# A fused attention, MLP and expert kernel: the second MLP matrix is split by GpSimd during the attention and kept in DRAM; the hash products and their transfers are regrouped

## Chip, cores and metric

The kernel runs on one core of one Trainium2 chip. The metric is the device time of one execution in microseconds (us). All arrays are float32 in DRAM.

## The reference

```python
# attention: 2 batches, 8 heads, 768 rows, head size 64; proj is 64 x 6
q_bits = (q @ proj > 0);  k_bits = (k @ proj > 0)              # 6 hash bits per row
mask   = bucket(q_bits)[:, None] == bucket(k_bits)[None, :]     # same bucket
scores = where(mask, q @ k.T / 8, -1e9)
attn   = exp(scores - max) / (sum + 1e-9);   x = attn @ v       # x: 1536 x 512
# MLP: w_in 512 x 2048, w_out 2048 x 512
h = x @ w_in
g = (a0 + a1 h + a2 h^2 + a3 h^3) / (1 + |b0||h| + |b1| h^2 + 1e-6)
x = g @ w_out
# experts: 8 of 512 -> 1024 -> 512; each row goes to its argmax expert
out[row] = gate * sigmoid_gate * (relu(x @ w1[e]) @ w2[e])
```

## The kernel before

There are 16 attention heads, worked off one after the other in six steps each (one step is 128 query rows); `PAIRS` = 8 loop turns hold two heads each, `par` 0 and 1, and buffers with two copies are indexed by `par`. Every engine has its own instruction stream, written out by hand, and the streams meet in semaphores. The steps of TensorE are in `step` (L515): it turns q and k of a head two ahead (`turn_qk`, L449, into the PSUM bank `ps_p`), multiplies them with the hash matrix (`hash_qk`, L462, into the same bank), computes scores for two steps ahead (`scores`, L470), transposes probabilities (`turn_probs`, L487) and multiplies them with v (`attend`, L499).

The mask is made by extra rows of the score product. `hash_qk` gives the projections and their negatives; VectorE compares and scales them (`mask_rows`, L1009, 128 x 384 into `mask_st`); SyncE copies 12 rows at a time from `mask_st` into rows 64 to 75 of `q_mask` and `k_mask` (`place_masks`, L293, four transfers for a head). The bank `ps_p` is free for the next `turn_qk` only when `mask_rows` has read it.

Products keep float32 accuracy by splitting each operand into a high part in the TensorE type float32r and a low part, and by three products (high-high, high-low, low-high). For q and k GpSimd makes the high part `qkT_hi` (L1347) and the low parts (L1354, L1360), and SyncE places the high part four times (`place_hi`, L287). GpSimd also splits one 128-column piece of `w_in` for each head (`split_win`, L1391), scales the attention output by the inverse row sums (L1381), which come back from DRAM as a broadcast row (`load_scale`, L312), and makes its low part (`lo_of_x`, L1383).

SyncE issues all transfers of the attention in the order of `attention_head` (L335): masks, inverse sums out, v, inverse sums in, a piece of `w_in`, q and k, x into `xT`, high parts. It waits before each one (`hold`, L258), so an issue that has to wait holds up all behind it.

The MLP has four groups of 384 rows and in each 16 pieces f of the 2048 hidden columns. TensorE alternates `mlp_up` (L577, 12 products) and `mlp_down` (L587, 9 products), three pieces apart; ScalarE and VectorE work out g between them, GpSimd its low part (L1460). In the first group there is more to do. `w_out` comes in 16 pieces of 128 x 512 into three buffers `x2_sb` (`load_wout`, L367); ScalarE makes the high part (`hi_of_wout`, L867), VectorE the low part (`lo_of_wout`, L1132), 16 pieces over the first ten steps (`TAIL` = 10), and each later load waits for a low part (L390). At step 4 ScalarE waits for the last transfers of x (L906), since `wout_hi` and `wout_lo` lie over buffers of the attention. The tile pool of the attention and that of the MLP share one stretch of SBUF.

After the MLP the rows are routed to experts, and 19 slots of 128 rows go through the expert matrices, which ScalarE, VectorE and GpSimd split in the same way.

## Time and profile before

| | us |
|---|---|
| median of 3 runs (821.36 to 823.01) | 822.98 |
| profiled execution, its own time | 822.91 |
| span of its trace, first to last instruction | 820.9 |
| TensorE busy | 785.3 (96%) |
| VectorE busy | 662.0 (81%) |
| ScalarE busy | 589.6 (72%) |
| GpSimd busy | 347.6 (42%) |

In the trace the attention lies from 0 to about 255 us, the MLP from 256 to about 550, the routing to about 575 and the experts to the end. PE is TensorE, PEld its weight loads, DVE is VectorE, ACT ScalarE, POOL GpSimd, SP SyncE. A busy TensorE need not be at its peak, since the ends of its products are modelled. "L583" is line 583 of the kernel. The column of the granted clock reads 1.00 for 2.4 GHz and 0.50 for 1.2 GHz.

### The profile page before, as it was taken

To read this page: it belongs to the slowest core of one execution; us is meant where nothing else is said; L and a number is where in the kernel's file an instruction comes from. 1 tells how busy PE (TensorE), PEld (TensorE's weight loads), DVE (VectorE), ACT (ScalarE), POOL (GpSimd) and SP (SyncE) were. 2 spreads that over 40 slices of the span, in tenths; PEclk is the share of its full clock that TensorE was granted. 3 is DMA by queue.
4 is the path that set the end of the run, shared out by engine and by line. 5 is a ranking of instruction groups with operands and counts; after the bars stand their busy time and mean duration, and the time that the engine had idled before them with its cause. 6 is when DMAs were issued, how large, how long until landed. Compare 5 with 4: busy or idle time off the path is not lost.

```text
span 820.9 us, 16572 instructions
## 1 busy us (share of the span) xinstructions
PE 785.3 (96%) x5050; PEld 678.1 (83%) x5050; DVE 662.0 (81%) x1101; ACT 589.6 (72%) x1046; POOL 347.6 (42%) x319
## 2 busy tenths in 40 slices
PE   8999999999998799999999999996999999999995
PEld 6888888888887688999899999976788888888884
DVE  5777777777785899788877878767899999999982
ACT  5666766767666688776676777642799988988973
POOL 5365565564643213222222222211356765565452
PEclk9999999999999999999999999997899999999999
DMA  5666786786644320100010010044782113516930
GB/s 128 141 149 159 164 180 145 174 179 146 157 98 117 109 77 2 39 1 0 0 38 0 0 38 0 1 142 165 273 288 80 38 51 111 170 45 213 373 124 1
DMA packets 75236, 88.64 MB, mean 108 GB/s; under 512 B 34355, under 2 KB 51459, under 8 KB 75204
## 3 DMA queue, kind: packets, MB, share of 16 engines
q1 hardware_dynamic: 72004, 80.11, 35.6%
q0 software_dynamic: 3040, 8.13, 3.0%
q8 instruction: 17, 0.28, 0.1%
q14 instruction: 15, 0.12, 0.1%
q10 hardware_dynamic: 160, 0.00, 0.0%
HBM read 108.82 MB, written 8.18 MB: 143 GB/s over the span
## 4 chain that ended last, share of the span: by engine, by line
PE 85%; DVE 7%; ACT 2%; issue 2%; DMA 2%; POOL 1%; DVEq 0%; SPq 0%; POOLq 0%; ACTq 0%
PE ps_s L583 14%; PE ps_t L751 13%; PE ps_s L728 13%; PE ps_t L601 9%; PE ps_o L510 9%; PE ps_t L496 7%; PE ps_o L601 4%; PE ps_s L481 4%; PE ps_s L483 3%; PE ps_s L737 2%; PE ps_p L459 2%; PE ps_p L466 1%; DVE mask_st L1014 1%; PE ps_o L715 1%; PE ps_p L642 1%
## 5 line engine op out<-in xcount | busy, mean ns | idle before, releaser
L1460 POOL TENSOR_TENSOR g_lo<-num_b,g_hi 128x384 fp32r<-128x384 f32 x64 | 65.8, 1028 | 217.3 <-ACT g_hi L875 128.1
L583 PE MATMUL ps_s<-xT,win_hi 128*128 (+1 forms) x512 | 133.0, 340 | 0.0
L1019 DVE TENSOR_REDUCE row_max<-ps_s 128x1 f32<-128x768 f32 x96 | 91.0, 948 | 44.9 <-PE ps_s L483 44.8
L1296 DVE TENSOR_TENSOR w_lo<-w_raw,w_hi 128x1024 fp32r<-128x1024 f32 x76 | 124.9, 1701 | 2.3 <-ACT w_hi L930 0.6
L795 ACT ACTIVATE probs<-ps_s,exp_bias,exp_scale 128x768 f32<-128x768 f32 x96 | 95.4, 993 | 9.1 <-DVE exp_bias L1031 8.9
L583 PEld LDWEIGHTS ps_s<-xT,win_hi 128*128 128x128 f32 x512 | 92.7, 189 | 3.8 <-issue 0.3
L801 ACT ACTIVATE probsT<-ps_t 128x384 f32<-128x384 f32 x96 | 47.3, 492 | 60.4 <-PE ps_t L496 60.4
L583 PE MATMUL ps_s<-xT,win_lo 128*128 (+1 forms) x256 | 86.2, 337 | 0.0
L496 PE MATMUL ps_t<-ident,probs 128*128 128x128 f32 x576 | 80.3, 276 | 0.9 <-DVE probsT L1045 0.9
L510 PE MATMUL ps_o<-probsT,v_raw 128*64 128x128 f32 x1152 | 76.3, 277 | 1.9 <-DVE probsT L1045 1.9
L930 ACT ACTIVATE w_hi<-w_raw 128x1024 fp32r<-128x1024 f32 x76 | 76.5, 1062 | 0.8 <-DMA w_raw<-in_moe_w_dram 0.6
L510 PEld LDWEIGHTS ps_o<-probsT,v_raw 128*64 128x64 f32 x1152 | 62.8, 137 | 16.9 <-issue 12.0
L938 ACT ACTIVATE w_hi<-w_raw 128x1024 fp32r<-128x1024 f32 x76 | 75.0, 1062 | 1.7 <-DMA w_raw<-in_moe_w_dram 1.6
L481 PE MATMUL ps_s<-k_mask,q_mask 76*128 76x384 f32 x192 | 73.8, 384 | 1.4 <-ACT qkT L790 0.9
L496 PEld LDWEIGHTS ps_t<-ident,probs 128*128 128x128 f32 x576 | 65.3, 140 | 8.1 <-issue 4.1
L1304 DVE TENSOR_TENSOR w_lo<-w_raw,w_hi 128x1024 fp32r<-128x1024 f32 x57 | 66.2, 1212 | 5.6 <-ACT w_hi L938 5.4
L1123 DVE SCALAR_TENSOR_TENSOR num_b<-num_b,coef,den_b 128x384 f32<-128x384 f32 x64 | 40.2, 629 | 32.9 <-ACT den_b L865 31.2
L483 PE MATMUL ps_s<-k_cross,q_cross 128*128 128x384 f32 x192 | 65.3, 340 | 0.0
L728 PE MATMUL ps_s<-w_hi,xgT_hi 128*128 128x512 f32 x152 | 61.7, 406 | 1.7 <-DVE xgT_lo L1309 1.7
L751 PE MATMUL ps_t<-w_hi,hT_hi 128*128 128x512 f32 x152 | 60.7, 399 | 1.2 <-issue 1.2
L1045 DVE COPY probsT<-ps_t 128x384 f32<-128x384 f32 x96 | 52.9, 551 | 9.9 <-PE ps_t L496 8.5
L728 PE MATMUL ps_s<-w_hi,xgT_lo 128*128 128x512 f32 x152 | 60.0, 395 | 0.0
(210 smaller groups left out, 1959.6 us busy)
## 6 DMA issues: line engine op xcount, KB each, us to landing
w_raw<-in_moe_w_dram SPq DMA_DIRECT2D x152, 512.0 KB
xT<-x_st SPq DMA_DIRECT2D x32, 192.0 KB, 3.7
scale_row<-row_inverse_scratch SPq DMA_DIRECT2D x32, 191.8 KB, 3.7
win_raw<-in_moe_w_in_dram SPq DMA_DIRECT2D x16, 256.0 KB, 3.9
x_sb<-in_moe_w_out_dram SPq DMA_DIRECT2D x16, 256.0 KB, 2.8
qk_raw<-in_q_dram SPq DMA_DIRECT2D x16, 192.0 KB, 3.2
qk_raw<-in_k_dram SPq DMA_DIRECT2D x16, 192.0 KB, 3.8
v_raw<-in_v_dram SPq DMA_DIRECT2D x16, 192.0 KB, 3.3
```

The lines of the kernel that those rows point to most:

```text
L481: pe.matmul(ps_s[slot][:, hb, 0:HALF], q_mask[par][0:KR, j * P:(j + 1) * P], k_mask[par][0:KR, cols], start=True, stop=False)
L483: mm = pe.matmul(ps_s[slot][:, hb, 0:HALF], q_cross[par][:, j * P:(j + 1) * P], k_cross[par][:, cols], start=False, stop=True)
L496: mm = pe.transpose(ps_t[hb][:, t * P:(t + 1) * P], probs[c % 2][:, col:col + P], ident[:])
L510: mm = pe.matmul(ps_o[g * D:(g + 1) * D, b * P:(b + 1) * P], v_raw[par][:, t, :], probsT[(QT * par + 2 * b + g) % 4][:, t, :], start=(t == ...
L583: mm = pe.matmul(h_bank[f % 4], a[w], xT[:, c, blocks, l, :], start=(c == 0 and n == 0), stop=(c == CD - 1 and n == 2))
L601: mm = pe.matmul(acc_bank[m][:], a[:, rows], b[:, f, :], start=(f == 0 and n == 0), stop=(f == NF - 1 and n == 2))
L728: mm = pe.matmul(h_slot[b], x[:, c, :], w[par][:, c, cols], start=(c == 0 and n == 0), stop=(c == CD - 1 and n == 2))
L751: mm = pe.matmul(y_ps[:], a[:, f, :], b[:, f, :], start=(f == 0 and n == 0), stop=(f == NE - 1 and n == 2))
L795: act.activation(probs[c % 2][:].rearrange("p (b n) -> p b n", b=2), ps_s[c % 2][:, :, 0:HALF], ACT.Exp, bias=exp_bias[:, c:c + 1], scale= ...
L930: act.activation(w1_hi[par][:, c, :], w1_raw[:, c, :], ACT.Copy).then_inc(w1_hi_made, 1)
L1019: dve.tensor_reduce(row_max[:, c:c + 1], ps_s[c % 2][:, :, 0:HALF], AX.XY, ALU.max).then_inc(maxed, 1)
L1296: dve.tensor_tensor(w1_lo[par][:, c, :], w1_raw[:, c, :], w1_hi[par][:, c, :].bitcast(F32), ALU.subtract).then_inc(w1_lo_made, 1)
```

## The change

Four edits.

- `w_out` is split during the attention. For each head SyncE loads one piece (`wout_raw`), GpSimd makes both parts (`split_wout`, at the end of its share of a head, before `lo_of_x`), and SyncE stores them, 512 KB, into a DRAM scratch. `hi_of_wout` and `lo_of_wout` are gone, and with them ScalarE's wait at step 4. SyncE loads the split pieces (512 KB each) into one tile `wout`: 0 and 1 when all scores are made, 2 to 5 after the place of the 15th head's x, 6 to 15 when all of x has been placed. `mlp_down` waits for piece f.
- The hash products of all heads but the first use a matrix of 32 columns and four groups of columns of the array, each on a quarter (192) of the rows. `mask_rows` then works on 128 x 192.
- The masks go through DRAM: one transfer out of `mask_st`, a wait until it has landed, and two transfers back (instead of four).
- The high part of k is placed into `k_mask` and `k_cross` by one transfer, since both now lie in one tile `k_both` (three transfers instead of four).

The first head keeps its own matrix `first_w` and its thresholds, so VectorE has more small instructions at the start.

```diff
@@ SyncE
+            def load_wout_raw(f):
+                sp.dma_start(wout_raw[:], wout_rows[f]).then_inc(wout_raw_in, 16)
+            def store_wout(f):
+                sp.dma_start(wout_dram[f], wout_st[:].bitcast(F32)).then_inc(wout_out, 16)
             def place_hi(par):
                 hi = qkT_hi[:].bitcast(F32)
-                for target, rows, part in ((k_mask, slice(0, D), slice(D, P)), (q_mask, slice(0, D), slice(0, D)),
-                                           (k_cross, slice(0, D), slice(D, P)), (q_cross, slice(D, P), slice(0, D))):
-                    sp.dma_start(target[par][rows, :].bitcast(F32), hi[part, :]).then_inc(hi_in[par], 16)
+                sp.dma_start(k_both[par][0:D, :, :].bitcast(F32),
+                             hi[D:P, :].unsqueeze(1).to_broadcast([D, 2, S])).then_inc(hi_in[par], 16)
+                for target, rows in ((q_mask, slice(0, D)), (q_cross, slice(D, P))):
+                    sp.dma_start(target[par][rows, :].bitcast(F32), hi[0:D, :]).then_inc(hi_in[par], 16)
+            def store_masks(par):
+                sp.dma_start(mask_dram[par], mask_st[:]).then_inc(mask_out, 16)
             def place_masks(par):
-                for hb in range(2):
-                    cols = slice(hb * HALF, (hb + 1) * HALF)
-                    for target, row in ((q_mask, HC * hb), (k_mask, HC * hb + ZK)):
-                        sp.dma_start(target[par][D:KR, cols].bitcast(F32),
-                                     mask_st[row:row + MR, :]).then_inc(mask_in[par], 16)
+                quarters = mask_dram[par].rearrange("(g r) n -> r g n", r=HQ)
+                for target, row in ((q_mask, 0), (k_mask, MR)):
+                    sp.dma_start(target[par][D:KR, :].bitcast(F32).rearrange("r (g n) -> r g n", n=QUARTER),
+                                 quarters[row:row + MR, :, :]).then_inc(mask_in[par], 16)
...
                     if more or par == 0:
                         hold(sp, masked, m + 2)
+                        store_masks(1 - par)
+                    if m0 > 1:
+                        hold(sp, wout_split, m - 1)
+                        store_wout(m - 2)
+                    load_wout_raw(m - 1)
+                    if more or par == 0:
+                        hold(sp, mask_out, 16 * (m + 1))
                         hold(sp, scored, QT * m)
                         place_masks(1 - par)
...
             def load_wout(f):
-                sp.dma_start(x2_sb[f % GT][:], wout_rows[f]).then_inc(wout_in[f % GT], 16)
+                sp.wait_ge(wout_out, 16 * (f + 1))
+                sp.dma_start(wout[:, f, :, :].bitcast(F32), wout_dram[f]).then_inc(wout_in[f], 16)
...
-            for f in range(GT):
+            sp.wait_ge(wout_split, NF - 1)
+            store_wout(NF - 2)
+            load_wout_raw(NF - 1)
+            sp.wait_ge(scored, QT * HEADS)
+            for f in range(2):
                 load_wout(f)
             sp.wait_ge(inverted, HEADS)
             store_inverse(1)
...
             load_scale(1)
+            sp.wait_ge(x_lo_made, START + HEADS - 1)
+            place_x(PAIRS - 1, 0)
+            for f in range(2, 6):
+                load_wout(f)
+            sp.wait_ge(wout_split, NF)
+            store_wout(NF - 1)
+            sp.wait_ge(x_lo_made, START + HEADS)
+            place_x(PAIRS - 1, 1)
+            sp.wait_ge(attended, BLOCKS * HEADS)
             for par in range(2):
-                sp.wait_ge(x_lo_made, START + HEADS - 1 + par)
-                place_x(PAIRS - 1, par)
-            for f in range(GT, NF):
-                sp.wait_ge(wout_lo_made, f - GT + 1)
+                sp.wait_ge(x_out[par], 16 * START + 32 * PAIRS)
+            sp.wait_ge(wout_out, 16 * NF)
+            for f in range(6, NF):
                 load_wout(f)
@@ TensorE
             def hash_qk(i, par):
                 pe.wait_ge(qk_copied, 4 * i + 2 * par + 2)
-                for hb in range(2):
-                    mm = pe.matmul(ps_p[HC * hb:HC * (hb + 1), 0:HALF], hash_w[:],
-                                   qkT[:, hb * HALF:(hb + 1) * HALF], start=True, stop=True)
+                for g in range(4):
+                    mm = pe.matmul(ps_p[HQ * g:HQ * (g + 1), 0:QUARTER], hash_w[:],
+                                   qkT[:, g * QUARTER:(g + 1) * QUARTER], start=True, stop=True)
                 mm.then_inc(hashed, 1)
...
-                pe.wait_ge(wout_lo_made, f + 1)
+                pe.wait_ge(wout_in[f], 16)
@@ ScalarE (mlp_step; hi_of_wout is gone)
-                if first:
-                    if f == 1:
-                        x_hi(PAIRS - 1, 1)
-                    if f == 4:
-                        for par in range(2):
-                            act.wait_ge(x_out[par], 16 * START + 32 * PAIRS)
-                    for b in range(NF * f // TAIL, NF * (f + 1) // TAIL):
-                        hi_of_wout(b)
+                if first and f == 1:
+                    x_hi(PAIRS - 1, 1)
@@ VectorE (lo_of_wout is gone)
-                dve.tensor_scalar(mask_st[:], ps_p[:, 0:HALF], hash_thr[:, 2:3], hash_thr[:, 3:4],
+                    dve.wait_ge(mask_out, 16 * (2 * i + par - 1))
+                dve.tensor_scalar(mask_st[:], ps_p[:, 0:QUARTER], hash_thr[:, 2:3], hash_thr[:, 3:4],
                                   ALU.is_ge, ALU.mult).then_inc(masked, 1)
@@ GpSimd
+            def split_wout(i, par):
+                n = 2 * i + par
+                pool.wait_ge(wout_raw_in, 16 * (n + 1))
+                if n > 0:
+                    pool.wait_ge(wout_out, 16 * n)
+                pool.tensor_scalar(wout_st[:, 0, :], wout_raw[:], 1.0, 0.0, ALU.mult, ALU.add).then_inc(wout_hi_made, 1)
+                pool.wait_ge(wout_hi_made, n + 1)
+                pool.tensor_tensor(wout_st[:, 1, :], wout_raw[:], wout_st[:, 0, :].bitcast(F32),
+                                   ALU.subtract).then_inc(wout_split, 1)
...
                     add_eps(i, par)
+                split_wout(i, par)
                 if 2 * i + par > 0:
                     lo_of_x(*done)
```

## Rows read from the trace of the kernel before

**Rows 1.** The page: the chain that ended last, by engine.
```profile
PE 85%; DVE 7%; ACT 2%; issue 2%; DMA 2%; POOL 1%; DVEq 0%; SPq 0%; POOLq 0%; ACTq 0%
```

**Rows 2.** Windows, a steady MLP stretch: length, busy by engine, clock, DMA share, GB/s.
```profile
350.00:400.00 50.00, 50.00 (x269) 45.55 (x268) 40.36 (x73) 34.64 (x72) 11.21 (x11) 1.00 0.00 0
```

**Rows 3.** Windows, one attention head of the loop.
```profile
98.19:113.33 15.14, 14.94 (x144) 12.64 (x146) 11.33 (x27) 10.51 (x23) 8.86 (x8) 1.00 0.71 166
```

**Rows 4.** Chain of waits within that head: start, length, what.
```profile
99.65 0.37 PE ps_s L481
100.02 0.18 PE ps_s L483
...
102.25 0.80 PE ps_p L466 x4
...
104.69 0.68 DVE mask_st L1014
```

**Rows 5.** Instruction groups by shape, 60 to 180 us: busy, mean ns, idle before.
```profile
L1399 POOL TENSOR_TENSOR win_lo<-win_raw,win_hi 128x512 fp32r<-128x512 f32 x8 | 10.3, 1294 | 0.7
...
L1025 DVE TENSOR_SCALAR exp_scale<-row_max 128x1 f32<-128x1 f32 x48 | 7.4, 154 | 1.7
...
L1014 DVE TENSOR_SCALAR mask_st<-ps_p,hash_thr 128x384 f32<-128x384 f32 x7 | 4.7, 669 | 0.0
```

**Rows 6.** Waits of the whole execution: us, times, longest.
```profile
PE ps_p L459 <- DVE mask_st L1014: 3.6, 14, 0.9
```

**Rows 7.** Waits of SyncE, 83 to 174 us (six heads).
```profile
SPq L261 <- PE ps_p L459: 6.9, 6, 1.6
```

**Rows 8.** Timeline of SyncE in that head: start, length, what.
```profile
106.40 0.65 SPq L291 DMA_DIRECT2D q_cross<-qkT_hi  x1
...
107.77 0.83 SPq L297 DMA_DIRECT2D q_mask<-mask_st  x1
...
110.21 0.71 SPq L297 DMA_DIRECT2D k_mask<-mask_st  x1
```

**Rows 9.** DMA issues of the whole execution: KB each, median us to landing.
```profile
x_sb<-in_moe_w_out_dram SPq DMA_DIRECT2D x16, 256.0 KB, 2.8
...
q_cross<-qkT_hi SPq DMA_DIRECT2D x15, 192.0 KB, 4.3
...
row_inverse_scratch<-row_inv SPq DMA_DIRECT2D x16, 3.0 KB, 1.6
```

**Rows 10.** Windows of 1 us, in that head and just before the MLP.
```profile
111.00:112.00 1.00, 1.00 (x12) 0.91 (x9) 0.85 (x4) 0.26 (x1) 0.00 (x0) 1.00 0.09 20
254.00:255.00 1.00, 0.78 (x7) 0.64 (x7) 0.30 (x2) 0.34 (x1) 0.00 (x0) 1.00 1.03 381
```

**Rows 11.** Timeline of GpSimd in that head.
```profile
114.71 1.01 POOL L1387 TENSOR_TENSOR x_st<-x_raw,x_st 128x384 fp32r<-128x384 f32 x1 [4.94 <-ACT x_st L812]
```

**Rows 12.** Timeline of TensorE in the first MLP group.
```profile
265.73 0.34 PE L583 MATMUL ps_s<-xT,win_lo 128*128 128x384 f32 x1
267.70 0.47 PE L601 MATMUL ps_t<-wout_hi,g_hi 128*128 128x512 f32 x1 [1.63 <-issue]
...
309.35 0.47 PE L601 MATMUL ps_t<-wout_hi,g_hi 128*128 128x512 f32 x1 [1.94 <-issue]
...
315.14 0.39 PE L601 MATMUL ps_t<-wout_hi,g_hi 128*128 128x512 f32 x1
```

**Rows 13.** Timeline of ScalarE at the same place.
```profile
264.86 1.16 ACT L870 ACTIVATE wout_hi<-x_sb 128x512 fp32r<-128x512 f32 x2
...
273.76 0.63 ACT L870 ACTIVATE wout_hi<-x_sb 128x512 fp32r<-128x512 f32 x1 [4.87 <-DMA x_sb<-in_moe_w_out_dram]
```

**Rows 14.** Timeline of GpSimd at the same place.
```profile
261.36 1.46 POOL L1381 TENSOR_TENSOR x_raw<-x_raw,scale_row 128x384 f32<-128x384 f32 x1 [4.20 <-DMA scale_row<-row_inverse_scratch]
```

**Rows 15.** Chain of waits in the steady MLP.
```profile
394.58 1.39 PE ps_t L601 x6
...
398.76 1.39 PE ps_t L601 x6
```

More of the change, by code:

```diff
@@ L97, in fused_kernel @@
                 row_inv = sb("row_inv", [P, STEPS])
-                k_cross = [sb(f"k_cross{i}", [P, S], F32R) for i in range(2)]
+                wout_raw = sb("wout_raw", [P, DM])
+                wout_st = sb("wout_st", [P, 2, DM], F32R)
                 v_raw = [sb(f"v_raw{i}", [P, QT, D]) for i in range(2)]
@@ L598, in mlp_down @@
                     rows = slice(m * P, (m + 1) * P)
-                    for n, (a, b) in enumerate(((g_hi[f % 4], wout_hi), (g_hi[f % 4], wout_lo),
-                                                (g_lo[f % 2], wout_hi))):
-                        mm = pe.matmul(acc_bank[m][:], a[:, rows], b[:, f, :], start=(f == 0 and n == 0),
+                    for n, (a, l) in enumerate(((g_hi[f % 4], 0), (g_hi[f % 4], 1), (g_lo[f % 2], 0))):
+                        mm = pe.matmul(acc_bank[m][:], a[:, rows], wout[:, f, l, :], start=(f == 0 and n == 0),
                                        stop=(f == NF - 1 and n == 2))
@@ L1003, in mask_first @@
                         rows = slice(row, row + MR)
[L1004 to L1006 removed]
+                        dve.tensor_scalar(target[0][D:KR, cols], ps_p[rows, 0:HALF], first_thr[rows, 2:3],
+                                          first_thr[rows, 3:4], ALU.is_ge, ALU.mult).then_inc(mask_in[0], 8)
+                dve.wait_ge(mask_in[0], 32)
                 dve.sem_inc(masked, 1)
@@ new lines, in _ @@
+            dve.tensor_scalar(hash_thr[0:HQ, 5:6], iota_p[0:HQ, :], float(MR), -BIG, ALU.is_ge, ALU.mult).then_inc(thr_made, 1)
+            dve.wait_ge(thr_made, 4)
+            dve.tensor_tensor(hash_thr[0:HQ, 2:3], hash_thr[0:HQ, 0:1], hash_thr[0:HQ, 1:2], ALU.add).then_inc(thr_made, 1)
+            dve.tensor_tensor(hash_thr[0:HQ, 3:4], hash_thr[0:HQ, 4:5], hash_thr[0:HQ, 5:6], ALU.add).then_inc(thr_made, 1)
+            dve.wait_ge(thr_made, 6)
+            for g in range(1, 4):
+                dve.tensor_copy(hash_thr[HQ * g:HQ * (g + 1), 2:4], hash_thr[0:HQ, 2:4]).then_inc(thr_made, 1)
@@ L1156, in mlp_step @@
                 from_hidden(g, f)
-                if first:
-                    for b in range(NF * f // TAIL, NF * (f + 1) // TAIL):
-                        lo_of_wout(b)
                 if not first and f in (4, 6, 8):
```

106 lines of the change are left out of this document (60 added, 46 removed).

## The prediction

> **What bounds the kernel now.** I read the page first: the chain that ended last runs through TensorE for 85% of the span, and TensorE is busy for 96% of it by the table [rows 1]. So an edit pays where TensorE waits, or where it takes work off TensorE. Next the windows, to see where it waits: in the steady MLP there is no idle time at all (50.00 of 50.00 us) and the DMA engines are at rest [rows 2]; nothing of the change touches that stretch. A head of the attention takes 15.14 us, TensorE is busy for 14.94 of them and the DMA engines for 71% [rows 3]: 0.20 us are to be had there, and the transfers have less room than any compute engine. Then the chain inside a head, to see what the 0.20 us are: the last non-TensorE piece of any length is the mask instruction on VectorE, 0.68 us, for which the next transposes into `ps_p` wait [rows 4]. Last, the first MLP group: only there does TensorE stand still for long.
>
> **Part 1: masks, VectorE.** The mask instruction took 669 ns on 128 x 384, and a tensor_scalar on 128 x 1 took 154 [rows 5]. Linear between them, 128 x 192 takes 154 + 192/384 x 515 = 412 ns, 0.26 us less, which is more than the 0.20 us that TensorE waits. All its waits for the mask are 3.6 us in 14 times [rows 6]; the longest, 0.9, is at the start and keeps about 0.6. Gain: 3.6 - 0.6 = 3.0 us.
>
> **Part 2: hash products, TensorE.** Four products' records (two halves, two passes each) take 0.80 us of the chain [rows 4]. They are now eight of half the length in four column groups. No row shows four groups at once, so I bound it. If all four stream together, the 0.64 us of pure streaming (4 x 384 columns at two cycles and 2.4 GHz, halved by the two groups; an estimate that fits the 0.80) becomes 0.32. If only two at a time do, nothing is saved. Against it stands a change of shape: the first score product after products with 64 columns takes 0.37 us in the chain, the next 0.18 [rows 4], so a change of the array's column split costs about 0.19 us. Before, the hash and the attention products behind it had the same 64 columns; now 32 meet 64, one such change more. Per head -0.32 + 0.19 = -0.13 to +0.19 us, for 15 heads -2.0 to +2.9. I take 0, near the middle, as no row is nearer to either end.
> The Trainium skill, TensorEngine Tiling (Array Packing), Key Properties, says that a change of tiling mode drains the engine while a change of tile does not, and its Theoretical Speedup gives up to four times for 32 columns. The 0.37 against 0.18 agrees with the first; the second no row here shows. By the speedup alone the sum would be 2 us lower, by the drain alone 2.9 higher.
>
> **Part 3: SyncE's queue in the attention.** Every transfer of a head hangs in one ordered queue. In six heads SyncE waited 6.9 us for TensorE's q/k transposes [rows 7], so it is spare for 1.15 us in each, and 0.95 once TensorE's head is 0.20 shorter. Gone are one issue of high parts, 0.65, and the four of masks, from 107.77 to 110.21 + 0.71 = 110.92, 3.15 us [rows 8]. New are three issues (masks out, split pair out, raw piece in), each between nearly nothing and the 0.83 of the dearest mask issue [rows 8], and a wait until the masks have landed in DRAM. Landing took 1.6 us for the 3 KB of inverse sums and 4.3 us for a high part behind three others [rows 9]. The mask store stands behind three high parts, so I take 3.3, and the other two issues lie inside it. Then two placements, 2 x 0.78. Sum: -0.65 - 3.15 + 3.3 + 1.56 = +1.06 us for a head, against 0.95 spare: SyncE would slip about 0.1 a head, 1.5 us over 14 heads. Ends: 1.6 gives -0.64, no slip; 4.3 gives +2.06, a slip of 1.1.
> A slip is hidden until it uses up the masks' lead. They are now issued by about 107.1 + 3.3 + 1.6 = 112.0 and land some 2 to 3 us later; the scores that need them stand just before the hash products, which come at 102.25 [rows 4] and one head later at 117.2, so at about 116.4. That is 1.4 to 2.4 us of lead, and a slip of 1.5 is just covered. I take off 0.5 for what is not.
> The data itself, 512 KB out and 256 KB in for a head, falls where the DMA engines now rest: they are 9% busy from 111 to 112 us [rows 10]. At the 381 GB/s of the wide raw pieces [rows 10] they are 2.1 us of data, and with the small pieces of the rest the engines' 71% [rows 3] become about 86%: it fits, with little left.
> The Trainium skill, DMA: Bandwidth & Descriptors, Anatomy of one DMA, puts most of about 2.0 us fixed cost on the receipt of the write. The 1.6 us for 3 KB is near it. By 2.0 instead of 3.3 SyncE would not slip, and the 0.5 would be gone.
>
> **Part 4: GpSimd.** The split adds a pair like that of `w_in`: 1.29 us for the subtraction [rows 5] and about half of that for the high part, 1.9 us. In each head GpSimd stood idle for 4.94 us before `lo_of_x` [rows 11], exactly where the pair is put; the raw piece, issued by about 109, should be there by 113, so the pair ends near 115 against 114.71. Behind the pair on GpSimd wait `lo_of_x` and the next head's high part, and for these SyncE's placements. By the spare time (4.94 - 1.9 = 3.0 us a head) the cost is 0; were the piece 3 us late, SyncE's queue would be late by what exceeds it.
>
> **Part 5: the first MLP group.** This is the large term. Before, `mlp_down` 0 starts at 267.70, 8 at 309.35, 9 at 315.14 [rows 12]. In between stand 16 high parts on ScalarE, 16 low parts on VectorE, ScalarE's wait for x and a raw piece, 4.87 us before 273.76 [rows 13], and a last raw piece before 309.35. All this goes. Then the group runs at TensorE's pace, one `mlp_down` after the other in 398.76 - 394.58 = 4.18 us [rows 15]; ScalarE is busy for 69% of such a stretch and VectorE for 81% [rows 2], so they keep up.
> The first `mlp_down`: one high part of `w_out` before the first logarithm and two (1.16 us [rows 13]) before g's high part fall away, about 1.3 us in the sum of both engines. TensorE itself is done with its four `mlp_up` at 265.73 + 0.34 = 266.07 [rows 12]. 267.70 - 1.3 = 266.4, held down by that to 266.3 at best; I take 266.3. The ninth after it starts at 266.3 + 9 x 4.18 = 303.9, against 315.14: 11.2 us. From the tenth on nothing is different.
> What is late next: the factors for the last head's x. GpSimd waited 4.20 us for them, to 261.36 [rows 14]; now 1.8 MB (a split pair out, a raw piece, two split pieces in) go into the queue ahead of them, against 0.77 MB before, 1.0 MB or 2.7 us more at 381 GB/s [rows 10], of which some 0.7 fall before the inverse sums are asked for. That puts them 2.0 us later, at 263.4; x is scaled 1.2 to 1.5 us later, at 264.7, and ScalarE asks for it at about 264.2. I take off 0.5. The split pieces 2 to 5 are there by 267, 6 to 15 are asked for at about 272 and come one in under 3 us, while TensorE needs number 6 at 266.3 + 6 x 4.18 = 291.4: hidden. TensorE's wait for all of x, at step 10, is 30 us away.
> The start: VectorE's additional small instructions lie in its waits for q, k and the constants. Cost 0, at most 0.4.
>
> **Sum.** -3.0 + 0.5 (masks and queue) + 0 (hash) - 11.2 + 0.5 = -13.2 us. Against the profiled execution's own 822.91 (its span is 820.9) that is 809.7; its time is within 0.1 us of the median 822.98. Forecast 809.7.
>
> **Rivals.**
> *A: the hash groups stream all at once and SyncE never slips.* For it: the landing of 1.6 us. Against: no row shows four groups. -3.0 - 2.0 - 11.2 = -16.2, so 806.7.
> *B: SyncE's queue sets the head in part.* Masks land in 3.8 us or issues cost 0.1 more each; slip 0.5 to 0.8 a head, less the lead of 1.7: 14 x 0.65 - 1.7 = 7.4 us back. With the two large gains, -3.0 - 11.2 + 7.4 = -6.8, about 816. For it: [rows 3, 7]; against: fewer small transfers in the DMA queue.
> *C: the queue turns the whole change over.* One mechanism: the wait for the masks in DRAM, with 512 KB and 256 KB behind it, makes SyncE's round longer than TensorE's head. It decides from a head of 15.14 + 11.0/14 = 15.9 us on, which is a round 1.0 us above TensorE's 14.94. With 4.3 us to landing, dear issues (0.83 each, within the wait) and the inverse sums' round trip longer by 0.7, a head takes 16.5: 14 x 1.36 - 11 = +8, so 831. Against: it needs all ends at once.
> *D: the first group gives half.* The factors or a split piece come 5 us late; ScalarE stands at step 1 or TensorE at an early `mlp_down`: 815. For it: the queue of 1.8 MB. Against: the lead of pieces.
> *E: the change does nothing, since the stall was TensorE's own.* [rows 12, 13] speak against; 823.
>
> **Chances.** Forecast 45% (its own range 807.5 to 812), A 17%, B 17%, C 8%, D 10%, E 3%. Range with both unknown ends: 805.5 to 818. What this kernel's measurement can tell from no change is about 0.2% (1.6 us). Faster: forecast, A, B, D, 89%, less 1 for their tails: 0.88; same 0.03; slower 0.09.
>
> **What would show it.** Head length: 14.9 to 15.0 right, above 15.14 B or C, and then TensorE waits for mask or high-part transfers at the first score product of a head. No wait for the mask instruction. The hash block in the chain: 0.55 to 0.7 is A, about 0.95 the drain alone. The tenth `mlp_down` 37.6 us after the first. No idle time of ScalarE for x in steps 1 to 4. What would make it wrong most cheaply: a mask store that lands more than 4 us after its issue.

## The result and the profile after

| | before | after |
|---|---|---|
| median of 6 runs each, interleaved, us | 822.62 (821.06 to 823.56) | 827.59 (826.19 to 828.24) |
| ratio after to before, 95% interval | | 1.0062 (1.0048 to 1.0076) |
| profiled execution, its own time | 822.91 | 828.0 |
| span | 820.9 | 826.2 |
| first `mlp_up` product starts | 255.80 | 265.93 |
| first `mlp_down` | 267.70 | 278.73 |
| tenth `mlp_down` | 315.14 | 317.91 |

The kernel became 0.62% slower where 1.6% faster was forecast. Between the two spans lie 5.3 us. The last three lines split them: the attention costs +10.13 (265.93 - 255.80). From the first `mlp_up` to the tenth `mlp_down` it is 51.98 us instead of 59.34, -7.36. Behind that nothing was expected, and +2.5 are there.

The page after: busy time by engine, the chain by engine, and the queue of SyncE's transfers (packets, MB, share of 16 engines).
```profile
PE 785.6 (95%) x5110; PEld 677.9 (82%) x5110; DVE 651.0 (79%) x1099; ACT 581.5 (70%) x1030; POOL 377.0 (46%) x351
...
q1 hardware_dynamic: 78892, 98.36, 42.2%
...
PE 73%; DMA 9%; SPq 8%; DVE 3%; issue 3%; ACT 1%; POOL 1%; POOLq 0%; DVEq 0%
```
TensorE's work is what it was (785.6 against 785.3 us), but its share of the chain fell from 85% [rows 1] to 73%, and DMA and SyncE's queue now hold 17%, where they had 2%. That is the first thing to see: the bound has moved to SyncE's ordered queue.

Two windows after: an early head (between two starts of `mask_rows`) and one of the middle.
```profile
72.67:87.42 14.75, 14.74 (x147) 12.51 (x147) 11.23 (x27) 10.51 (x23) 9.74 (x11) 1.00 0.85 206
103.53:119.66 16.13, 15.01 (x147) 12.55 (x147) 11.32 (x27) 10.51 (x23) 10.83 (x11) 1.00 0.92 207
```
A head takes 14.75 us up to the fifth, 0.39 less than before [rows 3], with TensorE busy throughout. From the sixth on the heads take 16.11, 16.13, 17.6, 15.38, 16.52, 16.36, 16.26, 19.45 and 14.75 us, and TensorE stands for 1.12 us in the one shown.

The chain inside such a head (start, length, what):
```profile
107.15 1.50 SPq L308
...
109.21 4.35 DMA hash_mask_scratch<-mask_st
...
114.19 1.91 DMA k_both<-hash_mask_scratch
116.09 0.34 issue
116.44 0.44 PE ps_s L531
...
117.40 0.46 PE ps_p L507 x8
```
TensorE's first score product waits for the placed mask, that for the mask in DRAM, and that for SyncE, which stood in the high part of q. Here is SyncE's round in the same head (start, length of the issue, what); it answers to [rows 8]:
```profile
105.85 0.60 SPq L305 DMA_DIRECT2D k_both<-qkT_hi  x1
106.50 0.60 SPq L308 DMA_DIRECT2D q_mask<-qkT_hi  x1
107.15 1.50 SPq L308 DMA_DIRECT2D q_cross<-qkT_hi  x1
109.21 0.34 SPq L311 DMA_DIRECT2D hash_mask_scratch<-mask_st  x1
109.91 0.46 SPq L301 DMA_DIRECT2D wout_split_scratch<-wout_st  x1
110.58 0.34 SPq L298 DMA_DIRECT2D wout_raw<-in_moe_w_out_dram  x1
113.82 0.31 SPq L316 DMA_DIRECT2D q_mask<-hash_mask_scratch  x1
114.19 0.36 SPq L316 DMA_DIRECT2D k_both<-hash_mask_scratch  x1
114.66 0.34 SPq L328 DMA_DIRECT2D row_inverse_scratch<-row_inv  x1
...
116.74 1.13 SPq L333 DMA_DIRECT2D scale_row<-row_inverse_scratch  x2
...
122.62 0.61 SPq L305 DMA_DIRECT2D k_both<-qkT_hi  x1
```
From 110.92 to 113.82 SyncE does nothing but wait. Through nearly all of this wait the DMA engines are full; they run low behind it, at the inverse sums (last two columns: DMA share, GB/s):
```profile
112.00:113.00 1.00, 1.00 (x20) 1.00 (x22) 0.93 (x4) 1.00 (x4) 0.00 (x0) 1.00 1.04 376
115.00:116.00 1.00, 0.31 (x3) 0.07 (x1) 0.93 (x4) 0.84 (x3) 0.62 (x1) 1.00 0.19 41
```
The round, from one high part of k to the next, is 16.77 us. For comparison the same four points of SyncE's round in the trace of before, where this one is 15.57 us (the rounds around it make up a mean head of 15.14):
```profile
104.44 0.50 SPq L291 DMA_DIRECT2D k_mask<-qkT_hi  x1
...
111.14 0.35 SPq L309 DMA_DIRECT2D row_inverse_scratch<-row_inv  x1
...
112.97 1.15 SPq L314 DMA_DIRECT2D scale_row<-row_inverse_scratch  x2
...
120.01 0.50 SPq L291 DMA_DIRECT2D k_mask<-qkT_hi  x1
```
After, the waits of SyncE over the attention (83 to 260 us: us, times, longest):
```profile
SPq L271 <- DMA hash_mask_scratch<-mask_st: 22.0, 10, 2.5
SPq L271 <- DMA row_inverse_scratch<-row_inv: 14.2, 12, 2.3
```
The wait for TensorE's transposes [rows 7] is gone: from 83 to 230 us SyncE waits for a compute engine only once, for 0.6 us (GpSimd), so it is practically never early any more. The landing times (KB, median us), for [rows 9]:
```profile
wout_split_scratch<-wout_st SPq DMA_DIRECT2D x16, 512.0 KB, 4.7
...
row_inverse_scratch<-row_inv SPq DMA_DIRECT2D x16, 3.0 KB, 1.9
...
q_cross<-qkT_hi SPq DMA_DIRECT2D x15, 192.0 KB, 5.9
```

The chain at the start of the MLP, which answers to [rows 12 to 14]:
```profile
265.59 4.49 DMA row_inverse_scratch<-row_inv
...
270.62 4.11 DMA scale_row<-row_inverse_scratch
...
274.87 1.63 POOL x_raw L1426
...
278.73 2.90 PE ps_t L650 x6
```
The factors of the last head come 13.5 us later than before (274.87 against 261.36), 3.4 of them beyond the 10.1 of the attention, and the first six products of `mlp_down` take 2.90 us instead of the 1.39 of [rows 15]. The windows say why (the column before the last two is the granted clock): 0.61 and 0.54, so about half of full speed (1.2 GHz), after TensorE had stood for 2.51 us before 278.73. Before the change it had stood there for 1.63 [rows 12] and ran on at 1.00.
```profile
278.00:280.00 2.00, 1.27 (x3) 1.11 (x4) 1.45 (x2) 1.93 (x4) 1.59 (x2) 0.61 1.03 354
280.00:282.00 2.00, 2.00 (x6) 1.52 (x6) 1.97 (x5) 0.84 (x2) 0.14 (x1) 0.54 0.98 330
```

### The profile page after: what moved, and what is told of

Read it like the earlier page. It is cut to its first block, busy times and chain, and to the rows that moved or that the text cites. A ratio compares the mean times of both kernels' runs of the same rounds, so it can differ in the third digit from the quotient of the medians.

```text
span 826.2 us, 16797 instructions
## 1 busy us (share of the span) xinstructions
PE 785.6 (95%) x5110; PEld 677.9 (82%) x5110; DVE 651.0 (79%) x1099; ACT 581.5 (70%) x1030; POOL 377.0 (46%) x351
## 4 chain that ended last, share of the span: by engine, by line
PE 73%; DMA 9%; SPq 8%; DVE 3%; issue 3%; ACT 1%; POOL 1%; POOLq 0%; DVEq 0%
PE ps_s L633 15%; PE ps_t L799 13%; PE ps_s L776 13%; PE ps_t L650 10%; PE ps_o L650 5%; DMA hash_mask_scratch<-mask_st 4%; PE ps_o L560 4%; PE ps_t L546 3%; DMA row_inverse_scratch<-row_inv 2%; SPq L308 2%; PE ps_s L531 2%; PE ps_s L785 2%; PE ps_s L533 2%; SPq L324 2%; PE ps_o L763 1%
## 5 line engine op out<-in xcount | busy, mean ns | idle before, releaser
L531 PE MATMUL ps_s<-k_both,q_mask 76*128 76x384 f32 x192 | 74.5, 388 | 12.3 <-DMA k_both<-hash_mask_scratch 9.3
L650 PE MATMUL ps_t<-wout,g_hi 128*128 128x512 f32 x248 | 78.1, 396 | 2.5 <-issue 2.5
L560 PE MATMUL ps_o<-probsT,v_raw 128*64 128x128 f32 x1152 | 78.0, 281 | 1.9 <-DVE probsT L1082 1.9
L533 PE MATMUL ps_s<-k_both,q_cross 128*128 128x384 f32 x192 | 65.6, 341 | 0.0
L902 ACT ACTIVATE den_b<-ps_s 128x384 f32<-128x384 f32 x64 | 31.3, 488 | 48.0 <-PE ps_s L633 47.8
```

What stands on the lines that cost most here:

```text
L531: pe.matmul(ps_s[slot][:, hb, 0:HALF], q_mask[par][0:KR, j * P:(j + 1) * P], k_mask[par][0:KR, cols], start=True, stop=False)
L533: mm = pe.matmul(ps_s[slot][:, hb, 0:HALF], q_cross[par][:, j * P:(j + 1) * P], k_cross[par][:, cols], start=False, stop=True)
L560: mm = pe.matmul(ps_o[g * D:(g + 1) * D, b * P:(b + 1) * P], v_raw[par][:, t, :], probsT[(QT * par + 2 * b + g) % 4][:, t, :], start=(t == ...
L650: mm = pe.matmul(acc_bank[m][:], a[:, rows], wout[:, f, l, :], start=(f == 0 and n == 0), stop=(f == NF - 1 and n == 2))
```

## The experiments

Theory Q: SyncE's round is one serial chain, and a DRAM write that is waited for lands only when the burst issued ahead of it (high parts, the 512 KB pair) has drained; the order of the transfers makes the head 16 us. Rival V: the added bytes alone do it, whatever the order. Rival P: it matters which queue issues. The expectations of the later runs call theory Q by the letter D. Times are medians; every kernel was compared with the kernel before in the same runs (there 822.3 to 822.8), and the ratio is to it.

**1. masks_only**: the masks through DRAM, the hash and `k_both`; `w_out` as before.
```diff
-                    if m0 > 1:
-                        hold(sp, wout_split, m - 1)
-                        store_wout(m - 2)
-                    load_wout_raw(m - 1)
```


> The hash, mask and high-part edits alone; w_out is split in the MLP as before. Theory Q (SyncE's round is one chain of issues and two DRAM round trips, and its length is the head): without the pair's issues and bytes ahead of them the masks land in about 3 us instead of 4.1 and SyncE fits; a head takes 14.74 us, as the first four heads of the changed kernel do, and the time is about 822.6 - 15 x 0.40 = 816.6. Theory V (the bytes of the split pair fill the DMA engines): the same, 816.6. If a head is above 15.1 here, the mask round trip alone is enough to lose.


Measured: 829.99, ratio 1.0111 (1.0080 to 1.0142). Heads 14.7 to 14.8 at first, then 15.3 to 17.8. The SyncE waits from 83 to 230 us:
```profile
SPq L269 <- DMA hash_mask_scratch<-mask_st: 34.5, 9, 5.6
SPq L269 <- DMA row_inverse_scratch<-row_inv: 6.6, 10, 1.3
```
Two issues of one round, and the DMA engines in between (last two columns: busy share, GB/s):
```profile
111.15 0.35 SPq L303 DMA_DIRECT2D hash_mask_scratch<-mask_st  x1
115.80 0.32 SPq L308 DMA_DIRECT2D q_mask<-hash_mask_scratch  x1
```
```profile
112.00:113.00 1.00, 1.00 (x9) 0.98 (x8) 0.52 (x2) 0.75 (x2) 0.00 (x0) 1.00 1.04 206
...
114.00:115.00 1.00, 1.00 (x21) 0.83 (x17) 0.78 (x3) 1.00 (x4) 0.04 (x1) 1.00 0.24 65
115.00:116.00 1.00, 1.00 (x9) 0.96 (x8) 0.03 (x1) 0.85 (x2) 0.96 (x1) 1.00 0.00 0
```
While the mask write is outstanding, the engines first work off the high parts at a share of 1.0 and then run empty, since SyncE issues nothing from 111.50 to 115.80. In this round burst and gap follow each other. The pair is not here at all, so its bytes are not needed for the loss; the DMA share from 83 to 230 us is 0.77, hardly above the 0.76 of before. Both theories had 816.6 for this run, and both missed it by 13 us: Q had let the masks land in about 3 us, and they took 4.3 (median).

**2. wout_only**: the pair through DRAM, the masks, hash and high parts as before (the diff's other edits undone).
```diff
+                    if m0 > 1:
+                        hold(sp, wout_split, m - 1)
+                        store_wout(m - 2)
+                    load_wout_raw(m - 1)
                     if more or par == 0:
                         hold(sp, masked, m + 2)
                         hold(sp, scored, QT * m)
                         place_masks(1 - par)
```


> The split of w_out during the attention alone; masks, hash and high parts as before. Theory Q: SyncE has 1.15 us to spare and gets two issues of about 0.45 with no wait for landing, so a head stays at 15.14; the first group gains 8 us as in the changed kernel: 814 to 815. Theory V: the 768 KB more in a head make it 15.8 or longer, and the time is 823 or more.


Measured: 828.76, ratio 1.0088 (1.0065 to 1.0111). Heads of 15.13 to 15.20 four times, then about 16. The write that is waited for is now that of the inverse sums, 3 KB, which lands in 2.7 us behind the pair instead of 1.6 [rows 9]:
```profile
SPq L265 <- DMA row_inverse_scratch<-row_inv: 13.4, 9, 2.9
```
So each of the two large parts, in the order that it had, loses by itself. The time falls into V's range (823 or more), not into Q's 814 to 815, which had left this wait out. This run alone doesn't tell the two apart: that the order and not the bytes makes the loss here too is shown only by run 10.

**3. overlap**: the inverse sums and v are issued between the mask store and the wait for it.
```diff
                     load_wout_raw(m - 1)
-                    if more or par == 0:
-                        hold(sp, mask_out, 16 * (m + 1))
-                        hold(sp, scored, QT * m)
-                        place_masks(1 - par)
                     hold(sp, inverted, m)
                     store_inverse(1 - par)
...
                         load_v(m + 1, 1 - par)
+                    if more or par == 0:
+                        hold(sp, mask_out, 16 * (m + 1))
+                        hold(sp, scored, QT * m)
+                        place_masks(1 - par)
```


> The changed kernel with SyncE's order in a head altered: inverse sums out and v in are issued while the masks are on their way to DRAM, and the masks are placed after them; all bytes are kept. Theory Q: both round trips run side by side, the round loses about 0.8 us of issues and 1.2 of waiting, and a head falls from 16.1 to between 14.74 and 15.1: 812 to 816. Theory V: the bytes are the same, a head stays near 16: 826 to 828.


Measured: 816.80, ratio 0.9936 (0.9912 to 0.9960). Heads about 15.4, SyncE's wait for the masks down to 4.0 us in 8 times, for the inverse sums 13.1 in 10. Two round trips laid over each other are worth 10.8 us against the changed kernel, with the same transfers and bytes (Q had 812 to 816, V 826 to 828). The inverse sums do not land sooner, they land later, 4.1 us (median) instead of 1.9: the gain is in what goes on meanwhile.

**4. scale_first**: at the end of the attention the inverse sums and their factors go ahead of the first two split pieces.
```diff
-            sp.wait_ge(scored, QT * HEADS)
-            for f in range(2):
-                load_wout(f)
             sp.wait_ge(inverted, HEADS)
             store_inverse(1)
             sp.wait_ge(inv_out, 16 * HEADS)
             sp.wait_ge(x_scaled, HEADS - 1)
             load_scale(1)
+            sp.wait_ge(scored, QT * HEADS)
+            for f in range(2):
+                load_wout(f)
```


> The changed kernel with the first two split pieces (1 MB) loaded behind the last inverse sums and factors instead of ahead of them. The inverse sums then land in 2 to 3 us instead of 4.5 and the first mlp_down starts 2 to 3 us sooner in both theories: 824.6 to 825.6; if the delay there has another cause, 827.6 stays.


Measured: 823.34, ratio 1.0015 (0.9998 to 1.0032). From the first `mlp_up` to the first `mlp_down` it is 10.8 us (265.63 to 276.42) instead of 12.8, and the six products take 1.63 us instead of 2.90:
```profile
276.42 1.63 PE ps_t L650 x6
```
The two together are 3.3 us, in the profiled executions; the medians, of two series, differ by 4.2, more than the 2 to 3 expected. The split pieces ahead of the factors had been the delay.

**5. masks_early**: masks_only with the mask store moved ahead of the high parts, so that the wait for it lies over their issue.
```diff
-                    if more or par == 0:
-                        hold(sp, masked, m + 2)
-                        store_masks(1 - par)
...
                 if more:
+                    hold(sp, masked, m + 3)
+                    store_masks(par)
                     hold(sp, qk_hi_made, m + 3)
                     hold(sp, scored, QT * (m + 1))
                     place_hi(par)
```


> The hash, mask and high-part edits alone, as in masks_only, but the mask store of a head is issued ahead of its high parts (0.77 MB) instead of behind them; SyncE waits for it one placement later. Theory D (SyncE waits for a small store that stands behind the burst it has just issued; the DMA engines run dry before it goes on, and burst plus gap is the head): the store has landed before it is waited for, a head falls from 16 to 14.74 us, 816 to 817. Theory V (the DMA engines have too much to do): the bytes and transfers are those of masks_only, a head stays at 16 and the time at 828 to 830.


Measured: 815.56, ratio 0.9923 (0.9902 to 0.9944), 14.4 us less than masks_only with the same bytes. All heads take 14.73 to 14.80 but the first; TensorE is busy for all of it, and the DMA share is 0.76:
```profile
102.18:116.92 14.74, 14.74 (x148) 12.49 (x147) 11.23 (x28) 10.53 (x23) 8.89 (x9) 1.00 0.76 176
```
The mask store and its placement: the three issues of high parts in between cover most of the round trip, and the write lands in 2.3 us (median) instead of 4.3.
```profile
102.74 0.35 SPq L303 DMA_DIRECT2D hash_mask_scratch<-mask_st  x1
...
104.65 1.30 SPq L300 DMA_DIRECT2D q_cross<-qkT_hi  x1
106.68 0.32 SPq L308 DMA_DIRECT2D q_mask<-hash_mask_scratch  x1
```
SyncE no longer waits for the mask write; it waits for the mask instruction of VectorE instead, 10.8 us in 10 times, and for TensorE again, 8.2 us in 7 times. This is the cleanest pair of the study: V gives the same time for both kernels, Q does not.

**6. early**: the whole change, with the edits of 4 and 5.


> The changed kernel with the mask store ahead of the high parts and with the two first split pieces loaded behind the last factors. Theory D: one of the two waits for a landing is gone, that for the inverse sums stays and stands behind 768 KB of the pair: a head of about 15.0 to 15.3, and with the first group's gain 809 to 814. Theory V: a head stays near 16 as in scale_first, 823.


Measured: 822.37, ratio 0.9992 (0.9976 to 1.0009). Heads about 16.1 still. The wait for the masks is gone, and that for the inverse sums takes its place:
```profile
SPq L271 <- DMA row_inverse_scratch<-row_inv: 21.4, 9, 3.0
```
They land in 3.3 us (median) with the pair issued ahead of them. The mask write, though it stands ahead of the high parts as in masks_early, takes 4.2 us here and not 2.3, so that place alone doesn't make it short. Taking away one wait showed the next of the same kind. By its number this run is V's (823), D had 809 to 814.

**7. early_pool**: early, with the pair's and the raw piece's transfers issued by GpSimd itself, not by SyncE.
```diff
+                pool.wait_ge(wout_split, n + 1)
+                pool.dma_start(wout_dram[n], wout_st[:].bitcast(F32)).then_inc(wout_out, 16)
+                if n + 1 < NF:
+                    pool.dma_start(wout_raw[:], wout_rows[n + 1]).then_inc(wout_raw_in, 16)
```


> As early, but GpSimd issues the pair out and the next raw piece itself, right after the split, on its own queue. Theory D: nothing of the pair stands in SyncE's queue, SyncE's round is about 12 us, a head 14.74, the last split piece is early: 805 to 809. Theory V: the same bytes on the same engines: a head of 15.5 to 16, 820. Against both: issuing two transfers costs GpSimd 1 us each, which its 3 us of spare time hold.


**8. wout_pool**: the same with wout_only.


> The split of w_out alone, as in wout_only, with the two transfers of a head issued by GpSimd. Theory D: the inverse sums no longer stand behind 768 KB in SyncE's queue and SyncE has two issues fewer, so a head is 15.14 again: 811 to 815. Theory V: 16 us as in wout_only, 828.


Measured: early_pool 820.17, ratio 0.9965 (0.9941 to 0.9989); wout_pool 823.11, ratio 1.0009 (0.9995 to 1.0022); of the ten runs of wout_pool one took 1290.94 at a granted clock of 0.56, where the others have 0.99; why is unexplained. Other queues give back 2 to 6 us, not the 11 to 15 of an order, and of wout_pool's part 4.1 us are in the first MLP group and only 2.8 in the attention (profiled executions, with 1.7 lost behind). early_pool's 820.17 is V's number (820), D had 805 to 809; wout_pool lies between D's 811 to 815 and V's 828. In early_pool SyncE's wait for the inverse sums was 33.1 us in 10 times, with a landing of 4.2, in a profile that is of the slowest of its ten runs (825.36). That fits a 3 KB write which stands behind the pair in the DMA engines, whoever issued the pair; it was not shown by itself. The two issues cost GpSimd 0.61 and 0.55 us each (medians), not 1. P falls as the main cause.

**9. regroup**: the inverse sums and v right behind the masks, then the pair and the raw piece (one head earlier), then the piece of `w_in`, and only then the wait for the inverse sums; with 4 and 5.
```diff
                         load_v(m + 1, 1 - par)
+                    hold(sp, wout_split, m)
+                    store_wout(m - 1)
+                    load_wout_raw(m)
...
+                if more or par == 0:
+                    load_win(m + 1, 1 - par)
+                if m0 > 0:
                     hold(sp, inv_out, 16 * m)
...
                     load_scale(1 - par)
```


> All bytes of the changed kernel, in an order in which no write that SyncE waits for stands behind a burst: masks out ahead of the high parts, inverse sums out and v in ahead of the pair, and between the inverse sums and the wait for them the pair and the piece of w_in; the raw piece is loaded one head earlier, so GpSimd does not wait for it. Theory D (waits for landings behind bursts are the whole loss): a head of 14.74 to 15.0 us, 804 to 809. Theory V (the 768 KB are too much for the DMA engines in any order): a head stays at 15.6 or above, 816 or more.


**10. wout_regroup**: the same order for wout_only.


> The split of w_out alone with the same order for the pair (behind the inverse sums and v, raw piece a head earlier) and the last factors ahead of the split pieces; masks, hash and high parts as before. Theory D: a head of 15.14, 809 to 813. Theory V: a head near 16, 822 to 828.


Measured: regroup 817.00 in 8 runs that spread from 807.21 to 820.73, ratio 0.9935 (0.9908 to 0.9963); wout_regroup 813.14, ratio 0.9885 (0.9859 to 0.9912), 15.6 less than wout_only, with all heads from the third on at 15.13 or 15.14 and the wait for the inverse sums at
```profile
SPq L265 <- DMA row_inverse_scratch<-row_inv: 1.7, 2, 1.1
```
The profiled execution of regroup is the one of 807.21, the fastest of the eight: ten heads of 14.74 to 14.76, with a DMA share of 1.01 from 95 to 155 us. The change can thus reach its forecast and pass it, but with the DMA engines full; by its median regroup is V's (816 or more), and D's (804 to 809) only in that one run. Even in that run SyncE waits 18.3 us in 10 times for the mask write, which lands in 4.9 (median), and the heads are short: a wait costs only by as much as it makes the round longer than TensorE's head. For wout_regroup the order theory had 809 to 813 and V 822 to 828. Of its gain, in the profiled executions, 9.7 us are in the attention and 5.0 in the first MLP group, where the last factors now go first. The inverse sums land in 2.7 us (median) as in wout_only; the wait is covered, not the landing shortened. Why the runs of regroup spread by 13 us was not settled; a share of 1.01 leaves nothing for a landing that is late once, which is an argument and not a measurement.

**11. late_scale**: `early`, with the wait for the inverse sums and their factors moved behind the loads of q and k.
```diff
-                    hold(sp, inv_out, 16 * m)
-                    if m0 > 1:
-                        hold(sp, x_scaled, m - 1)
-                    load_scale(1 - par)
...
                     load_qk(m + 4, par)
+                if m0 > 0:
+                    hold(sp, inv_out, 16 * m)
+                    if m0 > 1:
+                        hold(sp, x_scaled, m - 1)
+                    load_scale(1 - par)
```


> As early (822.4, a head of 16.2), but SyncE waits for the inverse sums only after it has issued the piece of w_in and q and k. Theory D: the waits of 21.4 us in 9 heads go, a head of 14.8 to 15.2: 806 to 812. Theory V: the wait goes elsewhere, a head stays near 16: 820 to 823.


Measured: 810.92 (810.01 to 812.01), ratio 0.9850 (0.9825 to 0.9874), 11.5 less than early, again with the same bytes. Heads 14.7 to 15.3, two of 16.08 and 15.73. SyncE's waits from 83 to 230 us:
```profile
SPq L271 <- PE ps_p L500: 9.9, 8, 2.2
SPq L271 <- DMA row_inverse_scratch<-row_inv: 5.3, 2, 3.0
```
SyncE is early again and waits for TensorE. The landing of the inverse sums is what it was, 3.4 us (median) against 3.3 in early; only the issues of q and k and of the piece of `w_in` now lie inside it. This version beats both kernels: the change with the mask store and the factors' loads moved takes 1.5% off the kernel before and 2.0% off the kernel after (810.92 / 827.59).

**12. early_half**: `early`, with half of the pair's bytes going out; the kernel leaves out the low part of `w_out` and reads the high part back in both places.
```diff
-                sp.dma_start(wout_dram[f], wout_st[:].bitcast(F32)).then_inc(wout_out, 16)
+                sp.dma_start(wout_dram[f], wout_st[:, 0:1, :].bitcast(F32)).then_inc(wout_out, 16)
...
-                sp.dma_start(wout[:, f, :, :].bitcast(F32), wout_dram[f]).then_inc(wout_in[f], 16)
+                sp.dma_start(wout[:, f, :, :].bitcast(F32), wout_dram[f].to_broadcast([P, 2, DM])).then_inc(wout_in[f], 16)
```


> As early, but only the high part of a piece is stored (256 KB instead of 512 KB in a head) and it is read back for both parts; the low part of w_out is left out. Theory V: two thirds of the added bytes less a head's wait, a head falls by about a third of the excess, from 16.2 to 15.7 or less: 815 or less. Theory D: the inverse sums still stand behind the pair, with 0.7 us less of data: a head of 15.6 and 815, so this run tells by how much bytes alone move a head with the order kept: if a head stays at 16.1 the bytes are not it.


Measured: 815.31, ratio 0.9910 (0.9882 to 0.9937), heads of 14.8 to 16.6 (15.6 on average from the fourth on), 7.1 us less than early. Both theories had 815, so the number doesn't choose between them. The bytes do count where the order is bad; that they count because the waited-for write stands behind them is the reading, not shown apart. V is right about the sign and wrong as a cause by itself: all bytes in another order (late_scale) did better than half of them in the old one.

**What they decide.** Four pairs with the same bytes differ by order alone: the changed kernel and overlap (10.8 us), masks_only and masks_early (14.4), early and late_scale (11.5), wout_only and wout_regroup (15.6, of which about 10 in the attention). The DMA share over the loop (83 to 230 us, or to 215 in the short runs) doesn't sort the heads either: masks_only 0.77 and masks_early 0.76, wout_only 0.87 and wout_regroup 0.99, early 0.88 and late_scale 0.92; in each of the last two pairs the faster kernel has the fuller engines. So V falls as a cause by itself. But the order theory as it was put down was too hopeful six times: masks_only, wout_only, early, early_pool, wout_pool and the median of regroup lie above its numbers, and in all but the first V's was the nearer or held. In the traces of the first five a wait for a landing was left (34.5, 13.4, 21.4, 33.1 and 23.6 us from 83 to 230 us). Of theory Q the serial round is shown. That the write lands only when the burst ahead of it has drained is borne out by masks_only against masks_early (4.3 and 2.3 us), but not by early (4.2 ahead of the high parts). How bytes and order add up to a head's length was not worked out.

## Why the prediction was wrong

**What bounds it** was read rightly as far as it went: TensorE's 0.20 us, and "the transfers have less room than any compute engine". The sum didn't use that second half enough.

**Part 1, masks on VectorE: right.** Predicted 412 ns, measured 469 (60 to 180 us, by shape), which is still 0.20 us less than the 669 of before, just the 0.20 us that TensorE had waited:
```profile
L1051 DVE TENSOR_SCALAR mask_st<-ps_p,hash_thr 128x192 f32<-128x192 f32 x7 | 3.3, 469 | 0.0
```
Heads that SyncE doesn't hold back have no idle time of TensorE (14.74 of 14.75 us).

**Part 2, hash: rival A's end, and a little past it.** Predicted 0, from bounds of -2.0 and +2.9. The eight records take 0.46 us in the chain instead of 0.80 [rows 4], 0.34 less, the 0.32 of all four groups streaming together. Head 14.74 against 15.14: 0.40 less, of which the wait had been 0.20 and the hash gives the other 0.20, about 3 us over 15 heads. The Trainium skill, TensorEngine Tiling (Array Packing), Theoretical Speedup, gives up to four times for 32 columns; the trace agrees with that, as twice as many groups took 0.46 us instead of 0.80. That 0.20 and not 0.34 arrive in the head leaves 0.14 at most for the added change of split; it was not measured by itself.

**Part 3, SyncE's queue: the step that failed.** The prediction put a head's round at +1.06 us against 0.95 spare, "SyncE would slip about 0.1 a head". In pieces of the round that is shown above, before [rows 8] and after:

| piece | predicted | measured |
|---|---|---|
| high parts up to the first mask issue | -0.65 | 3.33 to 3.36, +0.03 |
| masks and pair, to the inverse sums' issue | -3.15 + 3.3 + 1.56 = +1.71 | 3.37 to 5.45, +2.08 |
| inverse sums, issue to issue of the factors | 0 | 1.83 to 2.08, +0.25; up to 3.3 in later heads |
| sum | +1.06 | +2.36 |

So +2.36 stand against 1.15 us of spare time before [rows 7]. Three sizes were off. The landing of the mask write was taken as 3.3, between 1.6 and 4.3, and the upper end was the fact: 4.35 here, and store to placement 3.5 to 5.1 over the heads (4.61 here). The nearest row was `q_cross`, with 4.3 behind three high parts, since the mask store stands in the same place; the mean with a 3 KB write that stands behind nothing had no ground. The saved issue of a high part saved nothing: the third one now takes 1.50 us, where the four had 0.50 to 0.73 each, so that the high parts' issues end 2.80 us after their start instead of 2.61. And the wait for the inverse sums, which has the pair ahead of it, was not in the sum at all. One term was too dear: the two placements took 0.31 and 0.36, not 0.78 each. Against TensorE's faster 14.74 (not 14.94) the nine rounds from 58.30 to 205.54, of 15.5 to 17.4 and 16.36 on average, are a slip of 1.6 a head, not 0.1; the whole attention comes to +10.1 us, where the prediction had -2.5. The lead of the masks was put at 1.4 to 2.4 us; from the issue of a placement to the next hash products it fell from 6.5 us (49.05 to 55.60) over 5.2 and 4.1 to 3.5 (97.70 to 101.20), so 3.0 us were used up before TensorE began to stand. The Trainium skill, DMA: Bandwidth & Descriptors, Anatomy of one DMA, puts most of about 2.0 us on the receipt of a write; it gives this for transfers that GpSimd issues, and here SyncE issues them. The 96 KB write ahead of the burst, in masks_early, took 2.3 and is near it; behind the burst it took 4.3, and ahead of it but with the pair in the round (early) 4.2, and there its 2.0 is no guide.

With that the case is rival C, "the wait for the masks in DRAM, with 512 KB and 256 KB behind it, makes SyncE's round longer than TensorE's head": 831 predicted at 8%, 827.6 measured. Its head of 16.5 us is the mean of the nine heads from the sixth on, but that the two times lie so near is luck in part: its sum has +19 us in the attention and -11 in the first group, and measured are +10.1, -7.4 and another +2.5 behind. "It needs all ends at once" was the fault in its chance. The ends are not independent: a long queue makes the landing of the masks, that of the inverse sums and the issue behind them long together. C was right in the mechanism, but masks_only shows that the 512 KB are not needed for it.

**Part 4, GpSimd: 0, held, but not as told.** The pair doesn't end near 115: the raw piece comes late, and GpSimd stands before it.
```profile
POOL wout_st L1453 <- DMA wout_raw<-in_moe_w_out_dram: 67.6, 16, 7.2
```
It cost no more than the idle time that was there: from 83 to 230 us SyncE waited for GpSimd once, 0.6 us. In late_scale the same wait is 36.3 us in 10 times from 83 to 230 us and the heads are short.

**Part 5, the first MLP group: right in kind, 3.3 us short** (7.36 of 11.2 - 0.5). The pace of 4.18 us is there from the second `mlp_down` on, and no split piece was late. The first starts 12.8 us after the first `mlp_up` instead of the predicted 10.5, 2.3 more, for the factors, for which 0.5 had been taken off. scale_first gives 2.0 of it back by order alone. The tenth follows after 39.2 us instead of 37.6, 1.6 more, at half clock, which the prediction had not: it put TensorE's stand at 0.3 us. 11.2 - 2.3 - 1.6 = 7.3, and 7.36 were measured.

**Behind the group**: +2.5 us, not predicted. The gather for the experts starts at 572.55 instead of 568.25, 4.3 later, where 2.8 were behind the group. It lands in 6.26 us instead of 5.58, and the last 0.3 follow. In the last group's `mlp_down` the granted clock is 0.66 from 550 to 555 us, where before it was 1.00 from 548 to 552, and its chain has
```profile
550.12 3.01 PE ps_t L664 x9
```
The change touches nothing there, and no experiment was aimed at it. From the tenth `mlp_down` to the end it is 505.8 us before and 508.3 after, but 505.8 in overlap, 505.6 in regroup, 506.8 in early and 511.3 in early_pool, which have the same code from there on. So these 2.5 us are not a fixed price of the change; one execution of each was profiled, and why the clock is granted otherwise stays open.

## What to carry to other kernels

In an ordered DMA queue, price a wait on a DRAM write by what is in flight with it, not by its own size, and add up every such wait and issue of the round: if the round is longer than the head of the busiest engine, it is the head. Put other issues between the write and the wait for it; with the same bytes this was worth 10.8, 14.4, 11.5 and 15.6 us here (5.0 of the last in the first MLP group). The landing itself became shorter only in masks_early. When several bounds of an estimate have one common cause (a full queue), take their ends together and not as independent.

## What the runs showed of the hardware

- The landing of the same 96 KB write (medians): 2.3 us ahead of the three high parts (masks_early), 4.3 behind them (masks_only); with the pair in the round as well, 4.1 behind them (the changed kernel), and ahead of them 4.2 (early), 3.4 (late_scale) and 4.9 (regroup).
- The three issues of high parts took 0.60, 0.60 and 1.50 us, the four smaller ones before 0.50, 0.59, 0.73 and 0.65: 2.80 against 2.61 from the first start to the last end. Over all heads the third has a median of 1.56 us, in masks_early 1.30. The engine of the queue seems to be held in the issue when much is outstanding; this was not measured by itself.
- Issuing a transfer of 12 mask rows took 0.71 to 0.87 us out of SBUF before and 0.31 to 0.37 out of DRAM after. But one of the two placements out of DRAM had a median of 0.89 us in masks_early, 0.90 in early and 1.00 in late_scale, so the source alone doesn't set it.
- Four groups of 32 columns of TensorE's array nearly halve the time of two groups of 64 in the chain: 0.46 against 0.80 us for the same rows. 0.20 us of it shortened the head.
